# Attention with an output gate: one reciprocal of (1 + exp(-o)) times the denominator on VectorE, and the y transposes moved behind the q and k transposes

## The chip, the core and the metric

The kernel runs on one core of one Trainium2 chip. Its time is device microseconds from one launch, and the number that counts is the median over several runs. One profiled execution gives the trace from which every row below is taken.

## The reference, cut to what matters

Three layers follow one another. Attention is the layer that is touched; the others are only named.

```python
# attention, for each batch b (2), head h (8) and step t (768), head_dim 40:
m_new  = max(f_gate + m, i_gate)
C      = exp(f_gate + m - m_new) * C + exp(i_gate - m_new) * outer(v, k)
n      = exp(f_gate + m - m_new) * n + exp(i_gate - m_new) * k
h      = C @ q
denom  = max(abs(n . q), 1)
o      = 1 / (1 + exp(-o_gate))
y      = o * h / denom
# x = y as (1536 tokens, 320); an MLP 320 -> 2048 -> 320 with leaky relu;
# then 8 experts 320 -> 1024 -> 320, every token through all of them, weighted by a
# normalised gate (8 rounds over rows and columns)
```

## The kernel before

The 768 steps are cut into 6 chunks of 128, and a **unit** is one chunk of one batch with its 8 heads: 12 units, numbered n = 0 to 11, batch n % 2. Units 0 and 1 are written out ahead, units 2 and 3 in a short unrolled loop, units 4 to 11 in a hardware loop of four units each turn. Every engine has a queue of its own written by hand, in order, and engines wait for one another by semaphores only. What sets the order around the change is therefore the order of calls in each engine's loop body.

For unit n, by engine:

- TensorE: `exponents(n)` builds the gate exponents in PSUM (L1073 to L1080); `inter(n-1)` multiplies q by the state (L1106); `transposes(n)` turns q and k (L1089), once `ws_done` says that the weighted scores of unit n-1 were read, for they share a bank; `intra_and_state(n-1)` multiplies the weighted scores by v (L1118, it signals `y_prod`) and k by the weighted v (L1126); `scores(n)` (L1096). `y_transposes(n-2)` (L1136, L1137) turns the finished y into the layout of the MLP; it waits for `yy_done` of its unit, and for `xlo_done` of the unit before it, because all units use the same bank `yt_ps`.
- ScalarE: `out_gate(n)` takes exp(-o_gate) into `eo` (L540), `high_parts(n-2)` copies the high part of the transposed y (L547, L548), `exponentials(n)` (L555), `qk_copies(n)` (L561 to L564), and in the hardware loop `high_piece` (L580, L582), the high part of a piece of the first MLP weights.
- VectorE: `finish_y(n-1)` (L836 to L847) joins both products into `hh`, takes the denominator into `den`, its reciprocal (L843, 8 numbers a partition), multiplies by the gate into `ug` (L844) and by `hh` into `yy` (L847). Then `weigh(n)` (L814), `new_state(n-1)` (L856), `sigmoid(n)` (the reciprocal of 1 + exp, 320 numbers a partition, L867) and `low_parts(n-1)` (L821, L822), the low part of the transposed y. `weigh(n)` stands behind `finish_y(n-1)` in the queue, and `finish_y(n-1)` starts when `y_prod` of unit n-1 is there.
- GpSimd: `one_plus(n)` adds 1 to `eo` (L456; for units 0 and 1 VectorE does it, L863), then `pool_unit(n)` (L466, L472), and in the hardware loop `low_piece` (L310 to L318), the low part of a piece of the weights.

After the loops TensorE transposes y of unit 10, does `inter(11)`, a first hidden group of the MLP (L1211), `intra_and_state(11)`, a second hidden group, transposes y of unit 11, and goes on with the MLP.

Of the kernel before, what the change touches and what calls it, by code (L numbers as in the profile page):

```python
# [20 lines left out]
F32 = mybir.dt.float32  # L21
F32R = mybir.dt.float32r
BF16 = mybir.dt.bfloat16
ALU = mybir.AluOpType
# [4 lines left out]
def at_least(eng, sem, count):  # L29

    if isinstance(count, int) and count <= 0:
        return
    eng.wait_ge(sem, count)


def build(nc, q, k, v, i_gate, f_gate, o_gate, w_in, w_out, w_gate, w1, w2, out):
    P = 128
    B, H, S, D = q.shape
# [7 lines left out]
    NU = NC * B  # L46
# [23 lines left out]
    U_IT = 4  # L70
# [6 lines left out]
    with ctx:  # L77
# [3 lines left out]
        def sem(name):  # L81
            return ctx.enter_context(nc.semaphore(name))
# [33 lines left out]
        def asb(name, shape, dt):  # L116
            return sb(name, shape, dt, attn)
# [29 lines left out]
        eo = [asb(f"eo{b}", [P, DM], F32) for b in range(B)]  # L147
        t1 = asb("t1", [P, H, DV], F32)
        hh = asb("hh", [P, H, DV], F32)
        den = asb("den", [P, 2, H], F32)  # L150
        sg = asb("sg", [P, H, D], F32)
        ug = asb("ug", [P, H, D], F32)
        yy = [asb(f"yy{b}", [P, H, D], F32) for b in range(B)]
        attn.close()
# [76 lines left out]
        eo_done = sem("eo_done")  # L231
# [5 lines left out]
        yy_done = sem("yy_done")  # L237
# [1 line left out]
        FIN = 5  # L239
        wv_done = sem("wv_done")  # L240
        sd_done = sem("sd_done")
        e1_first = sem("e1_first")
        e1_done = sem("e1_done")
        sg_done = sem("sg_done")
        raw_in = sem("raw_in")
        RAW_IN = 5 * 16
        w_high = sem("w_high")
# [80 lines left out]
        def unit(i, j):  # L328

            n = 4 * i + j  # L330
            return n, 2 * i + j // 2, j % 2
# [57 lines left out]
        def _(pool):  # L389
# [57 lines left out]
            def alone():  # L447

                pool.sem_inc(pool_waits, 1)

            def one_plus(i, j):

                n, c, b = unit(i, j)
                pool.wait_ge(eo_done, n + 1)
                alone()
                pool.tensor_scalar(eo[b][:], eo[b][:], 1.0, None, ALU.add).then_inc(e1_done, 1)  # L456

            def pool_unit(i, j):

                n, c, b = unit(i, j)  # L460
# [38 lines left out]

            pool.wait_ge(gates_ok, 2)  # L500
            for j in range(2, U_IT):
                one_plus(0, j)
                pool_unit(0, j)

            pool.wait_ge(wg_in, 48)
# [2 lines left out]
            pool.tensor_tensor(wg[:, :, E:2 * E], wg_raw[:], wg[:, :, 0:E].bitcast(F32), ALU.subtract).then_inc(wg_step, 1)  # L508
            with pool.Fori(1, NU // U_IT) as i:
                for j in range(U_IT):  # L510
                    one_plus(i, j)
                    pool_unit(i, j)
                    low_piece(pool, 0, 0, (i - 1) * U_IT + j)

# [18 lines left out]
        def _(act):  # L533
            def out_gate(i, j):

                n, c, b = unit(i, j)
                act.wait_ge(unit_in[j], 80 * (i + 1))

                at_least(act, sg_done, n - 1)
                act.activation(eo[b][:], og[j][:], ACT.Exp, scale=-1.0).then_inc(eo_done, 1)  # L540

            def high_parts(i, j):

                m, c, b = unit(i, j)
                act.wait_ge(e_done, m + 1)
                tok = bass.ds(c * L + b * S, L)
                act.copy(xh[:, :, tok], yt_ps[:, 0:KT, :])  # L547
                act.copy(xr[0:DR, tok], yt_ps[0:DR, KT, :]).then_inc(xhi_done, 1)  # L548
# [17 lines left out]
            def act_unit(i, j):  # L566

                out_gate(i, j)
                high_parts(i, j - 2)
                exponentials(i, j)  # L570
                qk_copies(i, j)

            def high_piece(s, par, n):

# [167 lines left out]
        def _(dve):  # L742
# [82 lines left out]
            def finish_y(i, j):  # L825

                n, c, b = unit(i, j)
                done = FIN * n

                def fin(ins, k):  # L830
                    ins.then_inc(fin_step, 1)
                    dve.wait_ge(fin_step, done + k)

                dve.wait_ge(y_prod, n + 1)
                r_col = rw_t[:, bass.ds(c * 48 + b * H, H)]
                fin(dve.tensor_tensor(t1[:], heads(inter_ps)[:, :, 0:DV],  # L836
                                      r_col.unsqueeze(2).to_broadcast([P, H, DV]), ALU.mult), 1)
                dve.tensor_tensor(hh[:], heads(intra_ps)[:, :, 0:DV], t1[:], ALU.add).then_inc(ysum_read, 1)
                dve.wait_ge(ysum_read, n + 1)

                fin(dve.tensor_scalar(den[:, 1, :], hh[:, :, D], -1.0, 1.0, ALU.mult, ALU.max), 2)
                fin(dve.tensor_tensor(den[:, 0, :], hh[:, :, D], den[:, 1, :], ALU.max), 3)
                fin(dve.reciprocal(den[:, 1, :], den[:, 0, :]), 4)  # L843
                fin(dve.tensor_tensor(ug[:], sg[:], den[:, 1, :].unsqueeze(2).to_broadcast([P, H, D]), ALU.mult), 5)  # L844

                at_least(dve, e_done, n - 1)
                dve.tensor_tensor(yy[b][:], hh[:, :, 0:D], ug[:], ALU.mult).then_inc(yy_done, 1)  # L847
# [8 lines left out]
                    last = dve.tensor_tensor(st[b][rows, :, e, 0:DV], sp_v[rows, :, e, 0:DV], sd[b][rows, :, e, 0:DV], ALU.add)  # L856
                last.then_inc(st_done, 1)

            def sigmoid(i, j):
                n, c, b = unit(i, j)  # L860
                if isinstance(n, int) and n < 2:
                    dve.wait_ge(eo_done, n + 1)
                    dve.tensor_scalar(eo[b][:], eo[b][:], 1.0, None, ALU.add).then_inc(e1_first, 1)  # L863
                    dve.wait_ge(e1_first, n + 1)
                else:
                    dve.wait_ge(e1_done, n - 1)
                dve.reciprocal(sg[:], eo[b][:].rearrange("p (h d) -> p h d", d=D)).then_inc(sg_done, 1)  # L867
                dve.wait_ge(sg_done, n + 1)


            weigh(0, 0)
            rest_rows(1)
            sigmoid(0, 0)
            finish_y(0, 0)

            dve.wait_ge(rw_exp, 3)
# [10 lines left out]
                    last = dve.tensor_copy(decp[rows, 1:NC, b, :], dec_all[rows, 1:NC, b, :, half])  # L887
            last.then_inc(gates_ok, 1)
            new_state(0, 0)
            sigmoid(0, 1)  # L890
            low_parts(0, 0)
            for j in range(2, U_IT):
                finish_y(0, j - 1)
                weigh(0, j)
                new_state(0, j - 1)
                sigmoid(0, j)
                low_parts(0, j - 1)
            with dve.Fori(1, NU // U_IT) as i:
                for j in range(U_IT):
                    finish_y(i, j - 1)  # L900
                    weigh(i, j)
                    new_state(i, j - 1)
                    sigmoid(i, j)
                    low_parts(i, j - 1)
            finish_y(NU // U_IT, -1)

            def leak(u, f):
# [160 lines left out]
        def _(pe):  # L1068
# [105 lines left out]
            for j in range(2, U_IT):  # L1174
                if j == 2:
                    pe.wait_ge(parts_ok, 2)
                exponents(0, j)
                if j == 2:

                    pe.wait_ge(gates_ok, 2)  # L1180
                y_transposes(0, j - 2)
                inter(0, j - 1)
                transposes(0, j)
                intra_and_state(0, j - 1)
                scores(0, j)
            with pe.Fori(1, NU // U_IT) as i:
                for j in range(U_IT):
                    exponents(i, j)
                    y_transposes(i, j - 2)
                    inter(i, j - 1)  # L1190
                    transposes(i, j)
                    intra_and_state(i, j - 1)
                    scores(i, j)

# [185 lines left out]
```

## Time and profile before

| | us |
|---|---|
| median of 3 runs | 1015.48 (1014.93 to 1016.15) |
| the profiled execution | 1015.77 |
| its span | 1014.0 |
| TensorE busy | 982.8 (97%) |
| VectorE busy | 461.9 (46%) |
| ScalarE busy | 299.6 (30%) |
| GpSimd busy | 93.7 (9%) |

The span goes from the first to the last instruction of the profiled execution. Busy shares are means over all of it: attention takes the first 128 us, where VectorE is the busiest together with TensorE, and the MLP and experts the rest, where TensorE is. Units follow one another in attention, so a time per unit counts up to twelve times.

### The profile page before, as it was taken

The page shows a single profiled execution, that of the slowest core. Times are in us where ns is not written, and L with a number is a line of the kernel's source. Part 1 is how long each engine was busy: PE and PEld are TensorE (multiplying, and loading weights), DVE is VectorE, ACT ScalarE, POOL GpSimd, SP SyncE. Part 2 cuts the span into 40 slices and gives each one's busy share as a digit, 9 for nine tenths or more (in the row PEclk, how much of TensorE's full clock was granted, in tenths as well). Part 3 has the DMA queues.
Part 4 walks back from the last instruction along what each step waited for, and adds up shares of the span by engine and source line. Part 5 has one row for each costly group of instructions (what it writes and reads, how often), then busy time and mean ns, then how long its engine had stood idle before and what let it go on. Part 6 is the DMA issues. An engine that isn't in the chain of part 4 may idle for free.

```text
span 1014.0 us, 15373 instructions
## 1 busy us (share of the span) xinstructions
PE 982.8 (97%) x5500; PEld 867.2 (86%) x5500; DVE 461.9 (46%) x818; ACT 299.6 (30%) x571; POOL 93.7 (9%) x159
## 2 busy tenths in 40 slices
PE   5899899999999989999999999999999999999998
PEld 4788778888778978988999999899999998899997
DVE  8999956645553255244244223424423332442222
ACT  5555334434442221132122112312212221221111
POOL 7456400000000323000000000000000000000000
PEclk8999999999999999999999999999999999999999
DMA  9665210030030003003000300300120030000000
GB/s 153 122 84 74 72 43 1 0 114 1 1 99 17 1 1 114 1 1 109 6 0 0 114 1 0 114 0 0 34 80 0 0 114 0 0 0 0 26 26 26
DMA packets 67168, 39.19 MB, mean 39 GB/s; under 512 B 51488, under 2 KB 63264, under 8 KB 67136
## 3 DMA queue, kind: packets, MB, share of 16 engines
q1 hardware_dynamic: 67136, 38.78, 16.6%
q8 instruction: 18, 0.29, 0.1%
q14 instruction: 14, 0.11, 0.0%
HBM read 36.81 MB, written 1.97 MB: 38 GB/s over the span
## 4 chain that ended last, share of the span: by engine, by line
PE 89%; DVE 9%; issue 1%; DVEq 0%; ACT 0%; POOL 0%; POOLq 0%; ACTq 0%
PE psA L1211 43%; PE psB L1249 11%; PE psB L1251 11%; PE psB L1250 11%; PE psB L1227 2%; PE psB L1229 2%; PE psB L1228 2%; DVE sg L867 2%; PE psB L1234 1%; PE psB L1233 1%; DVE ug L844 1%; DVE ws L814 1%; PE psB L1118 1%; PE psA L1096 1%; DVE t L836 1%
## 5 line engine op out<-in xcount | busy, mean ns | idle before, releaser
L973 DVE SCALAR_TENSOR_TENSOR gl<-psA,gh 128x512 fp32r<-128x512 f32 x192 | 132.8, 692 | 341.2 <-ACT gh L708 341.1
L708 ACT ACTIVATE gh<-psA 128x512 fp32r<-128x512 f32 x192 | 115.0, 599 | 537.9 <-PE psA L1211 537.9
L1249 PE MATMUL psB<-w2s,gh 128*128 128x320 f32 x768 | 237.6, 309 | 0.0
L1250 PE MATMUL psB<-w2s,gh 128*128 128x320 f32 x768 | 237.3, 309 | 0.0
L1251 PE MATMUL psB<-w2s,gl 128*128 128x320 f32 x768 | 237.2, 309 | 0.0
L1211 PE MATMUL psA<-xh,w1h 128*128 (+1 forms) x480 | 190.6, 397 | 0.0
L1211 PE MATMUL psA<-xl,w1h 128*128 (+1 forms) x480 | 189.8, 395 | 0.0
L1211 PE MATMUL psA<-xh,w1l 128*128 (+1 forms) x480 | 189.1, 394 | 0.0
L1250 PEld LDWEIGHTS psB<-w2s,gh 128*128 128x128 f32 x768 | 144.3, 188 | 5.5
L1249 PEld LDWEIGHTS psB<-w2s,gh 128*128 128x128 f32 x768 | 144.2, 188 | 5.1
L1251 PEld LDWEIGHTS psB<-w2s,gl 128*128 128x128 f32 x768 | 144.4, 188 | 0.0
L1211 PEld LDWEIGHTS psA<-xl,w1h 128*128 128x128 f32 x480 | 90.3, 188 | 21.0
L1211 PEld LDWEIGHTS psA<-xh,w1h 128*128 128x128 f32 x480 | 90.4, 188 | 15.9
L1211 PEld LDWEIGHTS psA<-xh,w1l 128*128 128x128 f32 x480 | 90.4, 188 | 15.7
L1211 PE MATMUL psA<-xr,w1l 128*128 (+1 forms) x240 | 94.7, 394 | 0.0
L1211 PE MATMUL psA<-xr,w1h 128*128 (+1 forms) x240 | 94.2, 393 | 0.0
L1018 DVE SCALAR_TENSOR_TENSOR acc<-psB,pg,acc 128x320 f32 (+1 forms) x84 | 40.4, 544 | 97.5 <-PE psB L1251 97.5
L1211 PEld LDWEIGHTS psA<-xr,w1l 128*128 128x128 f32 x240 | 45.1, 188 | 10.9
L1211 PEld LDWEIGHTS psA<-xr,w1h 128*128 128x128 f32 x240 | 45.2, 188 | 10.3
L909 DVE SCALAR_TENSOR_TENSOR leaky<-hs 128x512 f32<-128x512 f32 x48 | 33.1, 691 | 43.2 <-ACT hs L646 43.0
L914 DVE TENSOR_TENSOR gl<-leaky,gh 128x512 fp32r<-128x512 f32 x48 | 33.2, 692 | 28.7 <-ACT gh L651 28.1
L646 ACT COPY hs<-psA 128x512 f32<-128x512 f32 x48 | 28.1, 586 | 58.6 <-PE psA L1211 53.8
(178 smaller groups left out, 970.6 us busy)
## 6 DMA issues: line engine op xcount, KB each, us to landing
raw<-in_moe_w_dram SPq DMA_DIRECT2D x16, 640.0 KB, 8.4
raw<-in_moe_w_dram SPq DMA_DIRECT2D x8, 1024.0 KB, 5.3
raw<-in_moe_w_dram SPq DMA_DIRECT2D x16, 256.0 KB, 6.1
raw<-in_moe_w_out_dram SPq DMA_DIRECT2D x4, 640.0 KB, 10.6
raw<-in_moe_w_in_dram SPq DMA_DIRECT2D x2, 1024.0 KB, 6.1
qs<-in_q_dram SPq DMA_DIRECT2D x12, 160.0 KB, 3.3
ks<-in_k_dram SPq DMA_DIRECT2D x12, 160.0 KB, 3.9
vz<-in_v_dram SPq DMA_DIRECT2D x24, 80.0 KB, 3.8
```

The costliest lines, as they stand in the source:

```text
L646: act.copy(hs[:, f % 2, :], h_ps[:, f % HB, :]).then_inc(hs_ok, 1)
L708: act.activation(gh[:, f % RING, :], h_ps[:, f % HB, :], ACT.Relu).then_inc(ghi_ok, 1)
L867: dve.reciprocal(sg[:], eo[b][:].rearrange("p (h d) -> p h d", d=D)).then_inc(sg_done, 1)
L909: dve.scalar_tensor_tensor(out=leaky[:, f % 2, :], in0=hs[:, f % 2, :], scalar=0.01, in1=hs[:, f % 2, :], op0=ALU.mult, op1=ALU.max).then_ ...
L914: dve.tensor_tensor(gl[:, f % RING, :], leaky[:, f % 2, :], gh[:, f % RING, :].bitcast(F32), ALU.subtract).then_inc(g_ready, 1)
L973: dve.scalar_tensor_tensor(out=gl[:, f % RING, :], in0=h_ps[:, f % HB, :], scalar=0.0, in1=gh[:, f % RING, :].bitcast(F32), op0=ALU.max, o ...
L1018: dve.scalar_tensor_tensor(out=dst, in0=y_ps[:, j, 0:DM], scalar=gate, in1=dst, op0=ALU.mult, op1=ALU.add).then_inc(o_read, 1)
L1211: last = pe.matmul(bank, lhs, rhs, start=n == 0, stop=n == total - 1)
L1227: pe.matmul(bank, wh, gh[:, slot, :], start=first, stop=False)
L1249: pe.matmul(bank, gh[:, slot, cols], W2S[par][:, f, 0, :], start=first, stop=False)
L1250: pe.matmul(bank, gh[:, slot, cols], W2S[par][:, f, 1, :], start=False, stop=False)
L1251: last = pe.matmul(bank, gl[:, slot, cols], W2S[par][:, f, 0, :], start=False, stop=end)
```

## The change

On VectorE `finish_y` now waits for `eo_done` of its unit, forms `dd = (eo + 1) * den` in one instruction, takes one reciprocal of its 320 numbers into `ug`, and multiplies by `hh` as before. The reciprocal of 8 numbers, the product `ug`, the whole of `sigmoid` with its call in each unit, and GpSimd's `one_plus` are gone, with three semaphores; ScalarE's `out_gate` waits for `yy_done` in place of `sg_done`. On TensorE `y_transposes(n-2)` moves behind `transposes(n)`, on ScalarE `high_parts(n-2)` behind `qk_copies(n)`, and on VectorE the low parts of a unit are taken one unit later.

```diff
--- before.py
+++ after.py
@@ -148,7 +148,7 @@
         t1 = asb("t1", [P, H, DV], F32)
         hh = asb("hh", [P, H, DV], F32)
         den = asb("den", [P, 2, H], F32)
-        sg = asb("sg", [P, H, D], F32)
+        dd = asb("dd", [P, H, D], F32)
         ug = asb("ug", [P, H, D], F32)
         yy = [asb(f"yy{b}", [P, H, D], F32) for b in range(B)]
         attn.close()
@@ -239,9 +239,6 @@
         FIN = 5
         wv_done = sem("wv_done")
         sd_done = sem("sd_done")
-        e1_first = sem("e1_first")
-        e1_done = sem("e1_done")
-        sg_done = sem("sg_done")
         raw_in = sem("raw_in")
         RAW_IN = 5 * 16
         w_high = sem("w_high")
@@ -448,13 +445,6 @@
 
                 pool.sem_inc(pool_waits, 1)
 
-            def one_plus(i, j):
-
-                n, c, b = unit(i, j)
-                pool.wait_ge(eo_done, n + 1)
-                alone()
-                pool.tensor_scalar(eo[b][:], eo[b][:], 1.0, None, ALU.add).then_inc(e1_done, 1)
-
             def pool_unit(i, j):
 
                 n, c, b = unit(i, j)
@@ -499,7 +489,6 @@
 
             pool.wait_ge(gates_ok, 2)
             for j in range(2, U_IT):
-                one_plus(0, j)
                 pool_unit(0, j)
 
             pool.wait_ge(wg_in, 48)
@@ -508,7 +497,6 @@
             pool.tensor_tensor(wg[:, :, E:2 * E], wg_raw[:], wg[:, :, 0:E].bitcast(F32), ALU.subtract).then_inc(wg_step, 1)
             with pool.Fori(1, NU // U_IT) as i:
                 for j in range(U_IT):
-                    one_plus(i, j)
                     pool_unit(i, j)
                     low_piece(pool, 0, 0, (i - 1) * U_IT + j)
 
@@ -536,7 +524,7 @@
                 n, c, b = unit(i, j)
                 act.wait_ge(unit_in[j], 80 * (i + 1))
 
-                at_least(act, sg_done, n - 1)
+                at_least(act, yy_done, n - 1)
                 act.activation(eo[b][:], og[j][:], ACT.Exp, scale=-1.0).then_inc(eo_done, 1)
 
             def high_parts(i, j):
@@ -566,9 +554,9 @@
             def act_unit(i, j):
 
                 out_gate(i, j)
-                high_parts(i, j - 2)
                 exponentials(i, j)
                 qk_copies(i, j)
+                high_parts(i, j - 2)
 
             def high_piece(s, par, n):
 
@@ -840,8 +828,11 @@
 
                 fin(dve.tensor_scalar(den[:, 1, :], hh[:, :, D], -1.0, 1.0, ALU.mult, ALU.max), 2)
                 fin(dve.tensor_tensor(den[:, 0, :], hh[:, :, D], den[:, 1, :], ALU.max), 3)
-                fin(dve.reciprocal(den[:, 1, :], den[:, 0, :]), 4)
-                fin(dve.tensor_tensor(ug[:], sg[:], den[:, 1, :].unsqueeze(2).to_broadcast([P, H, D]), ALU.mult), 5)
+                dve.wait_ge(eo_done, n + 1)
+                fin(dve.scalar_tensor_tensor(out=dd[:], in0=eo[b][:].rearrange("p (h d) -> p h d", d=D), scalar=1.0,
+                                             in1=den[:, 0, :].unsqueeze(2).to_broadcast([P, H, D]),
+                                             op0=ALU.add, op1=ALU.mult), 4)
+                fin(dve.reciprocal(ug[:], dd[:]), 5)
 
                 at_least(dve, e_done, n - 1)
                 dve.tensor_tensor(yy[b][:], hh[:, :, 0:D], ug[:], ALU.mult).then_inc(yy_done, 1)
@@ -856,21 +847,8 @@
                     last = dve.tensor_tensor(st[b][rows, :, e, 0:DV], sp_v[rows, :, e, 0:DV], sd[b][rows, :, e, 0:DV], ALU.add)
                 last.then_inc(st_done, 1)
 
-            def sigmoid(i, j):
-                n, c, b = unit(i, j)
-                if isinstance(n, int) and n < 2:
-                    dve.wait_ge(eo_done, n + 1)
-                    dve.tensor_scalar(eo[b][:], eo[b][:], 1.0, None, ALU.add).then_inc(e1_first, 1)
-                    dve.wait_ge(e1_first, n + 1)
-                else:
-                    dve.wait_ge(e1_done, n - 1)
-                dve.reciprocal(sg[:], eo[b][:].rearrange("p (h d) -> p h d", d=D)).then_inc(sg_done, 1)
-                dve.wait_ge(sg_done, n + 1)
-
-
             weigh(0, 0)
             rest_rows(1)
-            sigmoid(0, 0)
             finish_y(0, 0)
 
             dve.wait_ge(rw_exp, 3)
@@ -887,21 +865,18 @@
                     last = dve.tensor_copy(decp[rows, 1:NC, b, :], dec_all[rows, 1:NC, b, :, half])
             last.then_inc(gates_ok, 1)
             new_state(0, 0)
-            sigmoid(0, 1)
-            low_parts(0, 0)
             for j in range(2, U_IT):
                 finish_y(0, j - 1)
                 weigh(0, j)
                 new_state(0, j - 1)
-                sigmoid(0, j)
-                low_parts(0, j - 1)
+                low_parts(0, j - 2)
             with dve.Fori(1, NU // U_IT) as i:
                 for j in range(U_IT):
                     finish_y(i, j - 1)
                     weigh(i, j)
                     new_state(i, j - 1)
-                    sigmoid(i, j)
-                    low_parts(i, j - 1)
+                    low_parts(i, j - 2)
+            low_parts(NU // U_IT, -2)
             finish_y(NU // U_IT, -1)
 
             def leak(u, f):
@@ -1178,17 +1153,17 @@
                 if j == 2:
 
                     pe.wait_ge(gates_ok, 2)
-                y_transposes(0, j - 2)
                 inter(0, j - 1)
                 transposes(0, j)
+                y_transposes(0, j - 2)
                 intra_and_state(0, j - 1)
                 scores(0, j)
             with pe.Fori(1, NU // U_IT) as i:
                 for j in range(U_IT):
                     exponents(i, j)
-                    y_transposes(i, j - 2)
                     inter(i, j - 1)
                     transposes(i, j)
+                    y_transposes(i, j - 2)
                     intra_and_state(i, j - 1)
                     scores(i, j)
```

## Rows read from the trace of the kernel before

**Rows 1.** Chain of waits of the first 170 us, summed by line.
```profile
by line: PE psA L1211 14.1%; DVE sg L867 10.2%; issue 6.5%; DVE ug L844 6.0%; DVE ws L814 5.0%; PE psB L1118 4.2%; PE psA L1096 4.0%; PE psB L1227 3.1%; DVE t L836 3.0%; DVE hh L838 3.0%; PE psB L1228 3.0%; PE psB L1229 2.9%; DVE rest L793 
```

**Rows 2.** Timeline, VectorE, one unit: start, length (us), engine, line, operation, tiles.
```profile
65.51 0.50 DVE L836 TENSOR_TENSOR t<-psB,rw_t 128x328 f32<-128x328 f32 x1
...
66.58 0.27 DVE L841 TENSOR_SCALAR den<-hh 128x8 f32<-128x8 f32 x1
...
67.08 0.20 DVE L843 RECIPROCAL den<-den 128x8 f32<-128x8 f32 x1
67.32 1.14 DVE L844 TENSOR_TENSOR ug<-sg,den 128x320 f32<-128x320 f32 x1
68.49 0.62 DVE L847 TENSOR_TENSOR yy<-hh,ug 128x320 f32<-128x320 f32 x1
69.03 1.21 DVE L814 TENSOR_TENSOR ws<-psA,ex 128x1024 f32<-128x1024 f32 x1
70.16 0.66 DVE L856 TENSOR_TENSOR st<-psB,sd 64x164 f32<-64x164 f32 x2
70.85 2.15 DVE L867 RECIPROCAL sg<-eo 128x320 f32<-128x320 f32 x1
73.17 0.42 DVE L821 TENSOR_TENSOR xl<-psB,xh 128x256 f32 x1 [0.17 <-DVE sg L867]
...
73.92 0.50 DVE L836 TENSOR_TENSOR t<-psB,rw_t 128x328 f32<-128x328 f32 x1
```

**Rows 3.** Timeline, TensorE, the same unit.
```profile
70.41 0.60 PE L1089 MATMUL psA<-ident,qs 128*128 128x128 f32 x4
...
71.29 1.92 PE L1118 MATMUL psB<-vz,ws 128*128 128x96 f32 x16
...
73.94 1.98 PE L1096 MATMUL psA<-qt,kt 128*128 128x128 f32 x16
```

**Rows 4.** Timeline, ScalarE and GpSimd, the same unit and the next.
```profile
68.07 1.25 POOL L456 TENSOR_SCALAR eo<-eo 128x320 f32<-128x320 f32 x1
...
70.11 0.26 ACT L548 CAST xr<-psB 64x128 f32 x1
...
73.16 0.51 ACT L580 CAST w1h<-raw  x1
...
74.25 1.00 POOL L310 TENSOR_TENSOR w1l<-raw,w1h  x1 [2.43 <-ACT w2s L582]
...
75.39 0.32 POOL L316 TENSOR_TENSOR w2r<-raw,w2s  x1
...
75.68 0.86 POOL L318 TENSOR_TENSOR w2s<-raw,w2s  x1
```

**Rows 5.** View of tile ug: times are min/median/max in ns.
```profile
L844 DVE TENSOR_TENSOR ug<-sg,den x12: 492/1134/1137, 32.3 to 126.5; 128x320 f32<-128x320 f32 x12
```

**Rows 6.** Timeline, VectorE and GpSimd, unit 1 finished and unit 2 weighed.
```profile
41.41 0.50 DVE L836 TENSOR_TENSOR t<-psB,rw_t 128x328 f32<-128x328 f32 x1 [1.15 <-PE psB L1118]
...
42.97 1.13 POOL L466 TENSOR_TENSOR wv<-vz,rw_t 128x164 f32<-128x164 f32 x2
43.12 0.66 DVE L844 TENSOR_TENSOR ug<-sg,den 128x320 f32<-128x320 f32 x1
...
44.37 1.21 DVE L814 TENSOR_TENSOR ws<-psA,ex 128x1024 f32<-128x1024 f32 x1
```

**Rows 7.** Busy time by stage: stretch, length, engines, granted clock, DMA share, GB/s.
```profile
30.00:36.00 6.00, 2.10 (x15) 1.49 (x16) 5.85 (x11) 1.44 (x3) 4.16 (x5) 0.92 0.97 212
```

**Rows 8.** Timeline of the last unit and the start of the MLP.
```profile
119.58 1.22 DVE L814 TENSOR_TENSOR ws<-psA,ex 128x1024 f32<-128x1024 f32 x1
...
119.72 0.44 PE L1136 MATMUL psB<-ident,yy 128*128 128x128 f32 x2 [1.56 <-DVE yy L847]
...
124.80 0.50 DVE L836 TENSOR_TENSOR t<-psB,rw_t 128x328 f32<-128x328 f32 x1 [0.36 <-PE psB L1118]
...
127.59 0.44 PE L1136 MATMUL psB<-ident,yy 128*128 128x128 f32 x2 [0.95 <-DVE yy L847]
```

## The prediction

> **What bounds the kernel now.** I read the page first, for which engine fills which part. TensorE is busy nearly throughout, and what the MLP and the experts take is untouched. So the question is when attention, whose last y is transposed at 127.59 us [rows 8], hands over. Next the chain of waits of the first 170 us, summed by line [rows 1]: outside the MLP's own lines the largest shares are VectorE's sigmoid reciprocal (10.2%) and the product `ug` (6.0%). Then VectorE's timeline of one unit [rows 2]: from one `t` to the next, 65.51 to 73.92, it never idles longer than the 0.17 us ahead of `xl`. A unit takes 8.43 us: the weighing starts at 69.03 in unit 5 and at 119.58 in unit 11 [rows 2, 8], 50.55 us for six units.
>
> The reader must then see a second thing in the same rows, in which order the waits end. Let T be the end of a weighing, 69.03 + 1.21 = 70.24. TensorE turns q and k from 70.41 and multiplies by v from 71.29 to 73.21 [rows 3]; before that nothing exists that `finish_y` could work on. VectorE fills just that gap: state to 70.82, sigmoid reciprocal to 73.00, low parts to 73.9, `t` at 73.92 = T + 3.68 [rows 2]. The reciprocal of 2.15 us is on the chain by the order of the queue, but TensorE would have held VectorE until T + 2.97 without it. Thus it costs 0.7 us of critical time there, not 2.15.
>
> The loop that must not grow is: weighing, turn q and k, multiply by v, `finish_y`, next weighing, since `weigh(n)` is queued behind `finish_y(n-1)`. Scores are no part of it: they begin at 73.94 and end at 75.92, the weighing they feed starts 8.43 us after 69.03, at 77.46 [rows 2, 3].
>
> **The change part by part, in a unit of the hardware loop.** All from T.
>
> Moved low parts and y transposes. Behind the weighing VectorE has state (to T + 0.58) and then low parts, 0.75 us with their gaps (73.17 to 73.92 [rows 2]): T + 1.35. They belong to unit n-3, whose high parts are long copied, so they don't wait. But the y transposes of n-2 write the bank that these low parts read, so TensorE, which has turned q and k by about T + 1.0, waits for T + 1.40. The transposes take about 0.4 us (0.44 for two matmuls [rows 8], the third overlapping), and the product with v is queued behind them: it starts at T + 1.8 in place of 1.05, ends 1.92 later at 3.7 [rows 3], and `t` starts at T + 3.75. That is 0.07 later than now, though VectorE has dropped 2.15 us from this gap: the reciprocal's absence turns into idle time of 2.4 us, from T + 1.35 to 3.75. The transposes' old wait for `yy` goes, but it was no delay: it lay beside the weighing.
>
> `finish_y`. `t` and `hh` take 1.07 with gaps (65.51 to 66.58 [rows 2]). The first `den` instruction took 0.27 and ended at 66.85, when GpSimd's `w1l` piece, which in this pattern starts 0.33 us behind `t` (74.25 beside 73.92) and runs 1.00, ended at 66.84 [rows 2, 4]: VectorE waits for GpSimd there. After the change that piece is later, since ScalarE copies the high parts of y, two copies of 0.26 and about as much, 0.5 us together, ahead of the weight piece of 73.16 [rows 4]: GpSimd starts at T + 4.01 + 0.5 less the 0.05 by which q and k are turned sooner, T + 4.45, and ends at 5.45. `den` wants to start at 3.75 + 1.07 = 4.82 and so ends at 5.5; bounds: 5.0 without the meeting, 5.5 with it. The second `den` instruction is 0.2 (66.88 to 67.08 by the start of the next row [rows 2]): T + 5.7.
>
> Out go the small reciprocal (0.24 from its start to the next) and `ug`; in comes `dd`. The trace has no `(a + 1) * b` over 128x320; the nearest row is `ug` itself, same operands and size, 0.492 at best and 1.137 where GpSimd is at work [rows 5]. The 1.14 arose beside the `w2s` piece: `ug` of 67.32 ended at 68.46, GpSimd's piece at about 68.1 [rows 2, 4]. In unit 2 `ug` was issued between the first and second of two GpSimd products and needed only 0.66 while GpSimd's pair stretched to 1.13 [rows 6], so VectorE gets in between two GpSimd instructions. `dd` at T + 5.7 falls on the 0.32 us piece ahead of `w2s`. I take 0.55; bounds 0.49, and 1.4 if it lands behind `w2s` (0.86 + 0.49, [rows 4, 5]). The wait for `eo_done` costs nothing: that exponential is made a unit earlier. Then the reciprocal over 320 numbers, 2.15 + 0.03: the same shape as the one removed. It goes to T + 8.45. `yy` follows; `weigh` starts 0.54 behind the start of `yy` (68.49 to 69.03 [rows 2]), about 0.41 when `yy` isn't stretched by `one_plus`, which is gone: T + 8.9.
>
> Sum: 3.75 to `t`, 5.15 from `t` to the weighing (before 3.52, 65.51 to 69.03), and 1.21: **10.1 us a unit in place of 8.43**. The 2.15 us moved from a stretch where TensorE's latency covered them into the one stretch that nothing covers.
>
> What else is removed: `sigmoid` 2.15 and its gap of 0.17, off the gap as said; `one_plus`, 1.25 us on GpSimd [rows 4], which waits 2.43 us for ScalarE in each unit anyway [rows 4], so nothing but the shorter `yy` counted above. The semaphores go with them. No DMA moves: the loads of a slot wait for `d_done` and `eo_done`, both earlier than needed.
>
> The whole. Start: unit 0 loses its sigmoid and its y transposes are out of the way of unit 1's products; by the order of the queues I get `t` of unit 1 1.1 us earlier than 41.41, at 40.3 (bounds: no gain, and 2.15). From there units 1 and 2 have no weight pieces beside them: 4.6 us from `t` to the weighing (1.07 + 0.4 + 0.52 + 2.18 + 0.41), so the weighing of unit 2 starts at 44.9 (now 44.37 [rows 6]); then 3.75 + 4.6 + 1.21 = 9.56 to unit 3 at 54.5, and 10.1 for each of units 4 to 11: 135.3 against 119.58 [rows 8], **+15.7**.
>
> The end: after the last weighing (T = 120.80 now) TensorE transposes y of unit 10 at 119.72, before T, because `yy` was enough. Now it waits for low parts to T + 1.40. What follows up to `t` of unit 11 took 124.80 - 119.72 = 5.08 [rows 8], so `t` is at T + 6.48 in place of 4.00. `finish_y` to the transposes of unit 11 took 2.79 (124.80 to 127.59); now 1.07 + 0.4 + 0.52 + 2.18 + 0.49 + 0.05 = 4.71. Together 11.19 against 6.79: **+4.4**. TensorE has only one hidden group of about 1.9 us to lay over it.
>
> Total 15.7 + 4.4 = 20.1. Behind attention TensorE is full, so nothing takes it back. The profiled execution's own 1015.77 (span 1014.0) becomes 1035.9; against the median, 1015.48, that is **1035.6**.
>
> **The rivals.** *One unit's VectorE work is the bound, and it shrinks (faster).* VectorE fills the unit, and by sums it loses 0.24, 0.17 and 0.65 (1.14 to 0.49), 1.06 of 8.43 us. If the 2.15 were as well covered as now, eight units give 8.5 and the start 1.1: 1006. It decides in this kernel by whether `weigh(n)` can pass `finish_y(n-1)`; it can't, as one queue holds both, and `t` needs the product with v. Even with no meeting of any kind and y transposes free, the loop is 2.9 + 4.6 + 1.21 = 8.7, above 8.43. The Trainium skill, "VectorE: DVE Perf Modes", section "Rules for kernel authors", advises for chained VectorE instructions to minimise their count, not their semaphores; this change takes one off each unit's chain, and by that rule alone the case here would come true. The rows above bear it out only as far as VectorE never idles. I give it 3 in 100, and no change 1.
>
> *VectorE and GpSimd don't meet.* `den` ends at T + 5.0 and `dd` takes 0.49: 9.56 a unit throughout, 8 times 0.55 less: 1031. For: pieces move with ScalarE, whose copies I place to a few tenths only. 21 in 100.
>
> *`dd` lands behind `w2s`.* 0.86 more in eight units: 1042.5. For: `ug` does just that now. Against: `dd` is issued 0.24 earlier in the row of pieces. 15 in 100.
>
> *TensorE's clock falls.* A unit leaves TensorE idle for some 2.2 us in one piece, and 2.8 at the end. In the trace it waits 1.56 us ahead of 119.72 [rows 8] with no drop, while in the stretch of 30 to 36 us, where it was busy for 2.10 of 6.00, the granted clock shows 0.92 [rows 7]. At the lower of the two levels, 1.2 against 2.4 GHz, the 3 us of TensorE work between T and `t` would take up to twice as long: 1045 to 1065 by how many units are hit. The Trainium skill, "TensorE: Matmul & The Clock Gate", section "Why this matters for your kernels", warns of idle gaps between bursts that send the clock back; by it this rival would be likelier the longer the gap. 8 in 100.
>
> **How the numbers follow.** Main case 52 in 100, with 1033 to 1039 for itself. The range of 1029 to 1044 takes in the second and third rivals and the bounds of the start, and leaves out the fall of the clock and the gain. What a measurement can tell is about 0.2%, 2 us: faster 0.03, the same 0.01, slower 0.96.
>
> **What would show it.** Right: from `t` to `ws` about 5.1 us and from `ws` to `t` about 5.0; VectorE idle for over 2 us ahead of `t`, released by the product with v; y transposes released by `xr` of the low parts; the last weighing near 135 us. `den` of nearly 0.7 us shows the meeting with `w1l`. Wrong: `t` to `ws` under 4 us, or a `dd` over 0.7, or a granted clock below 1.00 in 50 to 130 us. The forecast falls as a whole if VectorE's idle time ahead of `t` is missing.

## The result, and the profile after

The changed kernel is slower: 1042.61 us (median of 4 runs, 1041.67 to 1043.82) against 1015.82, a ratio of 1.0264 (95% interval 1.0247 to 1.0282), 26.8 us. The forecast was 1035.6, slower, with a range of 1029 to 1044.

The page of the changed kernel, its span and the busy time of each engine (us, share, instructions):

```profile
span 1040.1 us, 15320 instructions
...
PE 992.2 (95%) x5489; PEld 874.3 (84%) x5500; DVE 452.1 (43%) x804; ACT 299.8 (29%) x571; POOL 83.9 (8%) x149
```

VectorE does 9.8 us less work than before and GpSimd 9.8 less, and the kernel is 26 us longer. So the time is not in the sum of what these two engines do. TensorE is busy for 9.4 us more with the same work, which fits the falls of its clock shown below. VectorE's timeline of one unit of the hardware loop after the change, as [rows 2] show it before (start, length in us, engine, line, operation, tiles; in brackets the idle time ahead and what ended it):

```profile
87.85 1.22 DVE L802 TENSOR_TENSOR ws<-psA,ex 128x1024 f32<-128x1024 f32 x1
88.98 0.66 DVE L847 TENSOR_TENSOR st<-psB,sd 64x164 f32<-64x164 f32 x2
89.67 0.42 DVE L809 TENSOR_TENSOR xl<-psB,xh 128x256 f32 x1
90.11 0.28 DVE L810 TENSOR_TENSOR xr<-psB,xr 64x128 f32 x1
92.98 0.50 DVE L824 TENSOR_TENSOR t<-psB,rw_t 128x328 f32<-128x328 f32 x1 [2.58 <-PE psB L1093]
...
94.04 0.48 DVE L829 TENSOR_SCALAR den<-hh 128x8 f32<-128x8 f32 x1
...
94.76 0.54 DVE L832 SCALAR_TENSOR_TENSOR dd<-eo,den 128x320 f32<-128x320 f32 x1
95.33 2.15 DVE L835 RECIPROCAL ug<-dd 128x320 f32<-128x320 f32 x1
97.52 0.49 DVE L838 TENSOR_TENSOR yy<-hh,ug 128x320 f32<-128x320 f32 x1
97.93 1.22 DVE L802 TENSOR_TENSOR ws<-psA,ex 128x1024 f32<-128x1024 f32 x1
```

The unit is 97.93 - 87.85 = 10.08 us. The reader is to see two things: the bracket at `t`, 2.58 us idle until TensorE's product with v (L1093) was there, and the reciprocal of 2.15 us behind it, between `t` and the next weighing. From `t` to the weighing it takes 4.95 us, before 3.52.

TensorE and GpSimd in the same unit, which answer to [rows 3] and [rows 4]:

```profile
90.54 0.41 PE L1111 MATMUL psB<-ident,yy 128*128 128x128 f32 x2 [0.26 <-DVE xr L810]
...
90.90 1.92 PE L1093 MATMUL psB<-vz,ws 128*128 128x96 f32 x16
...
93.50 0.99 POOL L307 TENSOR_TENSOR w1l<-raw,w1h  x1 [2.86 <-ACT w2s L570]
...
94.91 1.11 POOL L315 TENSOR_TENSOR w2s<-raw,w2s  x1
...
99.30 0.63 PE L1064 MATMUL psA<-ident,qs 128*128 128x128 f32 x4 [1.97 <-DVE ws L802]
```

The y transposes wait for `xr` of the low parts, the product with v starts at 90.90, 1.83 us behind the weighing's end at 89.07 (before 1.05), and ahead of the next q and k transposes TensorE is idle for 1.97 us.

That idle time is the second part of the result. Five stretches of 2 us of the changed kernel (length, then busy time of PE, PEld, DVE, ACT, POOL with instructions, granted clock, DMA share, GB/s), and below them the end of attention as in [rows 8]:

```profile
48.00:50.00 2.00, 2.00 (x11) 1.96 (x10) 0.00 (x0) 1.66 (x5) 0.19 (x1) 0.50 0.00 0
58.00:60.00 2.00, 2.00 (x10) 2.00 (x11) 1.11 (x4) 1.07 (x2) 0.83 (x1) 0.50 0.04 8
90.00:92.00 2.00, 1.74 (x17) 1.53 (x15) 0.38 (x2) 1.83 (x5) 0.64 (x1) 1.00 0.00 0
110.00:112.00 2.00, 2.00 (x11) 1.96 (x10) 0.64 (x2) 0.99 (x3) 0.83 (x1) 0.50 0.00 0
142.00:144.00 2.00, 2.00 (x10) 1.97 (x11) 0.58 (x2) 0.53 (x2) 0.00 (x0) 0.50 0.99 234
```

```profile
139.24 1.22 DVE L802 TENSOR_TENSOR ws<-psA,ex 128x1024 f32<-128x1024 f32 x1
...
141.94 0.66 PE L1111 MATMUL psB<-ident,yy 128*128 128x128 f32 x2 [5.10 <-DVE xr L810]
...
149.25 0.50 DVE L824 TENSOR_TENSOR t<-psB,rw_t 128x328 f32<-128x328 f32 x1 [5.13 <-PE psB L1093]
...
153.99 0.69 PE L1111 MATMUL psB<-ident,yy 128*128 128x128 f32 x2 [2.90 <-DVE yy L838]
```

Four of the five show 0.50, the lower of the clock's two levels, with TensorE fully busy. Where it stays at 1.00, a unit of the hardware loop takes 10.09 us. Where it falls, `t` comes later behind the end of the weighing: 5.4 us in unit 2, 5.1 in unit 3 and 5.0 in unit 8, against 3.9 in units 4 to 7, 9 and 10; and in unit 11 8.8, where the forecast had 6.5. The y of unit 11 is transposed at 153.99, before at 127.59 [rows 8]: 26.4 us, the whole difference. From there on both kernels take 886 us to their end.

### The profile page after: what moved, and what is told of

The parts are those of the page before. It is cut to its first block, busy times and chain, and to the rows that moved or that the text cites. A ratio compares the mean times of both kernels' runs of the same rounds, so it can differ in the third digit from the quotient of the medians.

```text
span 1040.1 us, 15320 instructions
## 1 busy us (share of the span) xinstructions
PE 992.2 (95%) x5489; PEld 874.3 (84%) x5500; DVE 452.1 (43%) x804; ACT 299.8 (29%) x571; POOL 83.9 (8%) x149
## 3 DMA queue, kind: packets, MB, share of 16 engines
HBM read 36.81 MB, written 1.97 MB: 37 GB/s over the span
## 4 chain that ended last, share of the span: by engine, by line
PE 88%; DVE 9%; issue 2%; DVEq 0%; ACT 0%; POOL 0%; POOLq 0%; ACTq 0%
PE psA L1186 42%; PE psB L1224 11%; PE psB L1226 11%; PE psB L1225 11%; DVE ug L835 2%; PE psB L1093 2%; PE psB L1202 2%; PE psB L1204 2%; PE psB L1203 2%; PE psB L1209 1%; PE psB L1208 1%; DVE dd L832 1%; PE psA L1064 1%; DVE hh L826 1%; DVE t L824 1%
```

## Experiments

Each was timed beside the kernel before on one chip; the ratio is to that. The column "unit" is the usual distance from one weighing to the next in the hardware loop at granted clock 1.00.

| run | unit, us | time, us | ratio (95% interval) |
|---|---|---|---|
| before | 8.43 | 1015.8 to 1016.5 | |
| the change | 10.09 | 1042.61 | 1.0264 (1.0247 to 1.0282) |
| e1 fusion only | 9.66 | 1036.21 | 1.0209 (1.0176 to 1.0243) |
| e2 move only | 8.86 | 1022.85 | 1.0066 (1.0044 to 1.0089) |
| e3 change, no reciprocal | 9.12 | 1023.78 | 1.0073 (1.0051 to 1.0095) |
| e5 change, TensorE kept busy | 10.09 | 1038.75 | 1.0220 (1.0197 to 1.0244) |
| e4 before, no sigmoid reciprocal | 8.43 | 1013.43 | 0.9970 (0.9958 to 0.9981) |
| e6 before, weight pieces gated | 7.55 | 1008.44 | 0.9928 (0.9910 to 0.9946) |
| e7 tanh | 8.43 | 1013.47 | 0.9968 (0.9954 to 0.9982) |
| e8 tanh and gate | 7.42 | 1006.36 | 0.9893 (0.9873 to 0.9913) |
| e9 fusion, gated and filled | 8.94 | 1027.29 | 1.0111 (1.0090 to 1.0131) |

### The two halves of the change

**e1**, the changed kernel with the three orders put back:

```diff
-                    inter(i, j - 1)
-                    transposes(i, j)
                     y_transposes(i, j - 2)
+                    inter(i, j - 1)
+                    transposes(i, j)
...
-                    low_parts(i, j - 2)
+                    low_parts(i, j - 1)
```

> Only the fusion: one product and one reciprocal in finish_y, no sigmoid, no one_plus, but y transposes, high parts and low parts in the order of before. Theory A (the 2.15 us reciprocal has moved from the gap that TensorE's transposes and product with v cover into the loop weighing, product with v, finish_y, next weighing, and the moved y transposes add a wait of 0.7 us to that loop): t comes about 3.0 us behind a weighing's end in place of 3.8, a unit of the hardware loop takes about 9.6 us (before 8.43, the whole change 10.09), the last weighing stands near 130 us, and the time is 1028 to 1033. Rival B (the move of the y transposes is what costs, the fusion is free or better, since VectorE has 1.06 us less to do in a unit): a unit of 7.4 to 8.4 us, and a time of 1007 to 1016.

The unit is 9.66 us, as theory A said to a tenth, and rival B falls: the fusion by itself makes the kernel slower. The time is 3 us above what I wrote, since the clock falls here too. A unit where TensorE stayed at 1.00 and the next (VectorE's `t` and `den`, TensorE's transposes of q):

```profile
79.21 0.50 DVE L824 TENSOR_TENSOR t<-psB,rw_t 128x328 f32<-128x328 f32 x1 [1.79 <-PE psB L1093]
...
80.28 0.85 DVE L829 TENSOR_SCALAR den<-hh 128x8 f32<-128x8 f32 x1
...
84.53 1.22 DVE L802 TENSOR_TENSOR ws<-psA,ex 128x1024 f32<-128x1024 f32 x1
...
84.67 0.44 PE L1111 MATMUL psB<-ident,yy 128*128 128x128 f32 x2 [2.03 <-DVE yy L838]
...
86.67 1.06 PE L1064 MATMUL psA<-ident,qs 128*128 128x128 f32 x4
...
90.52 0.50 DVE L824 TENSOR_TENSOR t<-psB,rw_t 128x328 f32<-128x328 f32 x1 [3.44 <-PE psB L1093]
...
95.81 1.22 DVE L802 TENSOR_TENSOR ws<-psA,ex 128x1024 f32<-128x1024 f32 x1
```

Behind an idle time of 2.03 us the transposes of q take 1.06 in place of 0.60, and `t` comes 4.8 us behind the weighing's end in place of 3.1. Units 4, 6 and 9 of this run were so, and the clock fell at its end too (0.57 from 136 to 140 us). `den` takes 0.85: with `t` earlier, it meets nearly the whole `w1l` piece on GpSimd, which started at 80.10 and took 1.00.

**e2**, the kernel before with only the orders of the change, and low parts ahead of the sigmoid:

```diff
                     new_state(i, j - 1)
+                    low_parts(i, j - 2)
                     sigmoid(i, j)
-                    low_parts(i, j - 1)
...
-                    y_transposes(i, j - 2)
                     inter(i, j - 1)
                     transposes(i, j)
+                    y_transposes(i, j - 2)
```

> Only the move: y transposes behind the q and k transposes, high parts behind the q and k copies, low parts one unit later and ahead of the sigmoid, which stays with its reciprocal, the small reciprocal, the product and one_plus. Theory A: the product with v waits for low parts and y transposes, but the sigmoid (2.15 us) now fills that time, so t is only 0.1 us later from a weighing's end; the weight pieces on GpSimd come 0.45 us later and hold den and ug a little longer; a unit takes 8.5 to 8.9 us. At the end y transposes of unit 10 wait about 2.6 us longer, with an idle TensorE of about 4 us and then a lower granted clock, 2 to 5 us in all. Time 1019 to 1025. Rival B (the move is what costs 1.7 us a unit): a unit near 10 us and 1033 to 1042.

As theory A had it: 8.86 us a unit. The end costs most of the rest in the trace: TensorE waits for low parts there, the clock falls to 0.50, and `t` of unit 11 comes 8.1 us behind the last weighing, before 4.0. (The traced execution took 1024.48, 1.6 us above the median, so its end may be costlier than the usual one.) So the move costs 0.43 us a unit alone (8.43 to 8.86) and 0.43 on top of the fusion (9.66 to 10.09); the fusion costs 1.23 either way. The halves add up. On top of the fusion the 0.43 is a difference of two: `t` comes 3.91 us behind the weighing's end in place of 3.12, and the way from `t` to the next weighing falls from 5.32 to 4.95, because `den` then meets less of the `w1l` piece.

### The reciprocal itself

**e3**, in the changed kernel, and **e4**, in the kernel before:

```diff
-                fin(dve.reciprocal(ug[:], dd[:]), 5)
+                fin(dve.tensor_tensor(ug[:], dd[:], hh[:, :, 0:D], ALU.add), 5)
```

```diff
-                dve.reciprocal(sg[:], eo[b][:].rearrange(...)).then_inc(sg_done, 1)
+                dve.tensor_scalar(sg[:], eo[b][:].rearrange(...), 1.0, None, ALU.mult).then_inc(sg_done, 1)
```

> The changed kernel with the reciprocal of dd left out: an addition of dd and hh of the same size stands in its place, so y is not the reference's. Theory A: finish_y gets shorter by 2.15 less 0.5 to 0.6, about 1.6 us, and since nothing covers it each unit gets shorter by just that: 10.09 becomes about 8.4 to 8.5 us; twelve units give 19 to 20 us, and TensorE's idle stretches shrink so that some of the lost clock comes back: 1016 to 1023. Rival B (y transposes behind low parts set the pace): a unit stays over 9.5 us, time over 1035.

> The kernel before with the reciprocal of the sigmoid left out (a multiplication by 1.0 of the same size in its place, so y is not the reference's). Theory A (the 2.15 us of the sigmoid lie in a gap of VectorE's critical chain that TensorE's product with v holds open anyway): t can come only 0.7 us sooner, and most of that is eaten by GpSimd's weight pieces, which start by ScalarE's clock: den waits for the piece of 1.00 us and ug for the one of 0.86, so a unit is 8.3 to 8.4 us in place of 8.43 and the time 1012 to 1017. Rival B (VectorE is the bound of a unit, each of its instructions counts): 1.8 us a unit, 995 to 1000.

In e4 the unit stays at 8.43, with 1.8 us of VectorE's work gone from each: in the hardware loop the sigmoid's reciprocal cost nothing. Of the 3 us of the run 1.7 are there when unit 4 is weighed (58.91 for 60.59), before the weight pieces begin, and none is added up to unit 11 (117.86 for 119.58). The other 1.3 us are no more than the spread of what follows attention, which took 884.8 to 886.5 us in the traces of all these kernels. In e3 the unit falls to 9.12, by 0.97 and not by the 1.6 that I wrote, and the time of 1023.78 is just above the 1016 to 1023 expected. The rows show what took the reciprocal's place, e4's first (VectorE, and the piece on GpSimd), then e3's:

```profile
75.77 1.21 DVE L814 TENSOR_TENSOR ws<-psA,ex 128x1024 f32<-128x1024 f32 x1
...
80.11 0.50 DVE L836 TENSOR_TENSOR t<-psB,rw_t 128x328 f32<-128x328 f32 x1 [1.31 <-PE psB L1118]
...
80.99 1.00 POOL L310 TENSOR_TENSOR w1l<-raw,w1h  x1 [2.39 <-ACT w2s L582]
...
81.18 0.84 DVE L841 TENSOR_SCALAR den<-hh 128x8 f32<-128x8 f32 x1
...
82.49 1.14 DVE L844 TENSOR_TENSOR ug<-sg,den 128x320 f32<-128x320 f32 x1
```

```profile
83.09 0.54 DVE L832 SCALAR_TENSOR_TENSOR dd<-eo,den 128x320 f32<-128x320 f32 x1
...
83.66 1.03 DVE L835 TENSOR_TENSOR ug<-dd,hh 128x320 f32<-128x320 f32 x1
...
84.72 0.63 DVE L838 TENSOR_TENSOR yy<-hh,ug 128x320 f32<-128x320 f32 x1
85.28 1.21 DVE L802 TENSOR_TENSOR ws<-psA,ex 128x1024 f32<-128x1024 f32 x1
```

In e4 `t` is 3.13 us behind the weighing's end in place of 3.68, and `den` then stands still for 0.84 until the `w1l` piece ends, in place of 0.27 [rows 2]. In e3 the addition with two tiles takes 1.03 where the same size takes 0.49 alone, and `yy` 0.63, beside GpSimd. GpSimd's pieces start by ScalarE's pace: `w1l` begins 5.22 us behind the start of the weighing in e4 (80.99 - 75.77) as in the kernel before (74.25 - 69.03 [rows 2, 4]), though `t` came sooner. What VectorE does not spend in the reciprocal it spends waiting for the pieces. For e3 this means that the instruction put in the reciprocal's place was itself held up, so its 0.97 us is less than what the reciprocal alone costs.

### The clock

**e5**: small products whose results nobody reads, called fillers below: 24 ahead of each unit's q and k transposes and, at the end, 70 and 40 ahead of the y transposes of units 10 and 11 (these two calls are not shown).

```diff
+            def filler(count, bank=None):
+                bank = psB[:, 1, HP * VP:512] if bank is None else bank
+                for _ in range(count):
+                    pe.matmul(bank, warm_up[:, 0:P], warm_up[:, 0:P], start=True, stop=True)
...
             def transposes(i, j):
+                if not (isinstance(n, int) and n < 2):
+                    filler(24)
```

> The changed kernel with 24 small bf16 products of 128 columns, whose results nobody reads, ahead of each unit's q and k transposes, 70 ahead of the y transposes of unit 10 and 40 ahead of those of unit 11: they stand where TensorE is idle (2.0 us a unit, 5.1 and 2.9 at the end). Theory C (the steady unit of 10.09 us is what the working gave, and the 7 us beyond the forecast of 1035.6 are the three stretches at granted clock 0.50, at 48 to 52 and 58 to 61 us, at 110 to 112, and from 140 us): the granted clock stays at 1.00 from 40 us on, the unit stays at 10.1 everywhere, and the time falls to 1035 to 1038. Rival D (those units are long because of their own waits, the clock is a by-product): the clock rises and the time stays at 1041 to 1044.

```profile
52.00:60.00 8.00, 7.16 (x77) 6.62 (x77) 6.66 (x11) 2.48 (x5) 1.75 (x3) 1.00 0.62 85
...
110.00:120.00 10.00, 9.05 (x94) 8.50 (x93) 7.24 (x12) 4.35 (x10) 4.20 (x7) 1.00 0.00 0
...
140.00:150.00 10.00, 9.35 (x85) 8.32 (x86) 5.46 (x10) 1.70 (x4) 0.00 (x0) 1.00 0.63 192
```

From 44 us on the clock is at 1.00, the units are 10.0 to 10.2 throughout, and `t` of unit 11 comes 6.52 us behind the weighing: the forecast had 6.48. The ratio falls from 1.0264 to 1.0220: 22.3 us above the kernel before (1016.44 on this chip), where the change was 26.8 above and the forecast without a fall of the clock was 20.1. The time of 1038.75 is a little above my 1035 to 1038. One part is the fillers' own: `t` of unit 1 is at 41.31 and not at 39.97, since 24 fillers stand ahead of it in TensorE's queue and take 2.18 us at 36.12, where the clock is low in both kernels (0.62 from 36 to 38 us). From `t` of unit 1 to `t` of unit 11 the changed kernel takes 109.28 us and e5 103.73. These 5.55 us are what the falls of the clock cost behind 40 us.

### The fused loop with nothing around it, and the meetings with GpSimd

**e9** is e1 with the gate of e6 and 24 fillers ahead of each unit's y transposes. **e6** is one line in the kernel before:

```diff
+                    pool.wait_ge(yy_done, 4 * i + j)
                     low_piece(pool, 0, 0, (i - 1) * U_IT + j)
```

> The fusion alone, as in the run with only the fusion, with every cost around it taken away: GpSimd's weight pieces start when yy is done, and 24 small bf16 products that nobody reads stand ahead of each unit's y transposes, so that TensorE is not idle while VectorE forms the reciprocal. Theory A: what stays is the loop itself, 3.1 us from a weighing's end to t, 4.6 from t to the next weighing, 1.22 for the weighing: 8.9 us a unit at granted clock 1.00, above the 8.43 of before, and with the later start of the MLP (+1.9 us in finish_y of unit 11, +1.2 for the last weight piece) 1022 to 1028. Rival B (it was the clock and the meetings with GpSimd that made the fused form slow): a unit of 8.4 us or less and a time of 1010 to 1017.

> The kernel before, but GpSimd begins the weight piece of unit n only when yy of unit n-1 is done, that is beside VectorE's weighing, state and sigmoid, which read PSUM or one tile and were never stretched, in place of beside den and ug. Theory E (the meeting with GpSimd costs 0.65 us in ug, 0.1 in den and 0.1 in yy per unit): ug takes 0.49 to 0.55, a unit 7.6 to 7.8 us, where TensorE's own work of the unit is the next bound; the last weight piece is 1.2 us later for the first hidden group; 1009 to 1013. Rival: the stretched ug is no part of what ends last, time 1015 to 1018.

e9 gives 8.94 us a unit with the clock at 1.00 from 44 to 120 us and `den`, `dd` and `yy` at their shortest (0.17, 0.49, 0.49): with clock and meetings out of the way the fused form is still above the 8.43 of before. Rival B falls. (At the very end of attention, 130 to 132 us, the clock fell to 0.50 in e9 too; the unit is free of that, the time is not.) e6 gives 7.55, a little better than the 7.6 to 7.8 expected, and is 0.72% faster than the kernel before, at 1008.44 for the 1009 to 1013 expected. So with the same gate in both, the fusion costs 1.39 us a unit (7.55 to 8.94). `ug` in e6, and where the piece has gone:

```profile
72.32 0.17 DVE L842 TENSOR_SCALAR den<-hh 128x8 f32<-128x8 f32 x1
...
72.96 0.49 DVE L845 TENSOR_TENSOR ug<-sg,den 128x320 f32<-128x320 f32 x1
...
73.90 1.22 DVE L815 TENSOR_TENSOR ws<-psA,ex 128x1024 f32<-128x1024 f32 x1
...
74.28 1.00 POOL L310 TENSOR_TENSOR w1l<-raw,w1h  x1 [2.63 <-DVE yy L848]
```

`ug` is 0.49 in place of 1.14 and `den` 0.17 in place of 0.27. VectorE still forms the sigmoid's reciprocal while TensorE multiplies by v, as before, and the piece on GpSimd now runs beside the weighing.

### A faster version

**e7** replaces the sigmoid by (1 + tanh(o/2)) / 2, so that `sigmoid` and `one_plus` go as in the change (not shown in the lines below); **e8** adds the gate of e6 to it:

```diff
-                act.activation(eo[b][:], og[j][:], ACT.Exp, scale=-1.0).then_inc(eo_done, 1)
+                act.activation(eo[b][:], og[j][:], ACT.Tanh, scale=0.5).then_inc(eo_done, 1)
...
+                fin(dve.scalar_tensor_tensor(out=ug[:], in0=eo[b][:]..., scalar=1.0, in1=den[:, 1, :]...,
+                                             op0=ALU.add, op1=ALU.mult), 5)
...
+                dve.scalar_tensor_tensor(out=yy[b][:], in0=hh[:, :, 0:D], scalar=0.5, in1=ug[:],
+                                         op0=ALU.mult, op1=ALU.mult).then_inc(yy_done, 1)
```

> The kernel before with no reciprocal over 320 numbers at all: ScalarE takes tanh(o/2) in place of exp(-o), ug = (tanh + 1) * reciprocal(den), yy = (hh * 0.5) * ug; sigmoid and one_plus are gone. Theory A: VectorE loses 2.3 us a unit, but in the gap, so t comes 0.7 us sooner and den and ug then wait for the weight pieces: 8.2 to 8.4 us a unit, 2 us gained at unit 0: 1010 to 1014. Rival B (VectorE's sum): 7.4 us a unit or less and 1003 to 1007.

> The tanh form and the gated weight pieces together. Theory A with E: both covers are gone, t comes about 3.0 us behind a weighing, t to weighing takes 2.6 to 2.9 us, and a unit is bound by TensorE at 7.4 to 7.7 us: 1006 to 1010, the fastest of all. If the gain of the two is no more than that of the gate alone, 1010 to 1013, TensorE was already the bound with the gate.

e7 takes out the large reciprocal and GpSimd's `one_plus`, and the unit is still 8.43, as in e4: it is the pieces that hold it. What it gains comes ahead of them: in the trace unit 4 is weighed 4.9 us earlier (55.73 in place of 60.59), and unit 11 still 4.9. With the gate too the unit is 7.42 and the time 1006.36, the fastest here, 1.07% below the kernel before. Both runs are within what theory A expected. TensorE is the bound there, but so it is in e6 already. One stretch of e6, then two of e8:

```profile
60.00:70.00 10.00, 9.95 (x93) 9.66 (x93) 9.48 (x17) 6.71 (x14) 7.37 (x14) 1.00 0.84 98
```

```profile
60.00:70.00 10.00, 9.95 (x93) 9.75 (x94) 5.97 (x15) 6.54 (x14) 5.03 (x9) 1.00 0.63 78
...
90.00:100.00 10.00, 9.95 (x93) 9.75 (x94) 6.25 (x16) 6.22 (x13) 4.72 (x9) 1.00 0.01 1
```

TensorE is busy for 9.95 of 10.00 us in both, before for 8.47 in this stretch. Most of the gain is the gate's (8.0 of the 10.1 us by the medians). Removing the reciprocal on top of it pays 2.1 us and 0.13 a unit, and without the gate 3.0 us and nothing a unit: in either case most of it is gained at the start.

## Why the prediction was right, and what it mis-sized

**The loop.** Right. It said 10.1 us a unit, built of 3.75, 5.15 and 1.21; measured are 3.91, 4.95 and 1.22, so two small misses cancel. Where the reciprocal stood it cost 0.7 us of critical time by the forecast, and nothing by e4, since the meetings with GpSimd take that too; the fusion costs 1.23 (e1).

**The moved low parts and y transposes.** Right as a mechanism, 0.07 us forecast against the 0.23 that `t` came later, and idle time of 2.4 against 2.58. But the forecast compared with the old kernel only; against the fusion alone the move costs 0.43 us a unit (e1), which its sum contains and no sentence named.

**`den` and `dd`.** Right: `dd` 0.54 for 0.55, `den` 0.48 for 0.68: the piece on GpSimd stood where placed (4.43 us behind the weighing's end for 4.45), and `t` was 0.16 late. Neither the rival without meetings (9.56 a unit) nor the one with `dd` behind `w2s` came about; in the latter's place the `w2s` piece took 1.11 in place of 0.86, so here GpSimd waited. The Trainium skill, "SBUF — State Buffer", section "SBUF: two separate sides", says that of a VectorE instruction with two inputs in SBUF and a GpSimd instruction that reads SBUF the one that starts first holds the ports they share for its whole length, and the other waits. The trace agrees in the order: `dd` started at 94.76 and `w2s` at 94.91. In the size it agrees roughly: `dd` then had 0.39 us to run, and `w2s` took 0.25 longer.

**The start.** `t` of unit 1 at 39.97 for 40.3, the weighing of unit 2 at 45.03 for 44.9. That these agree is partly luck: the forecast had 4.6 us from `t` to the weighing in units 1 and 2, and they took 5.06 and 4.96.

**The end.** The step said 11.19 us from the last weighing's end to the y transposes of unit 11; it took 13.53. `finish_y` was right (4.74 for 4.71). What failed is the step that what follows the y transposes, up to `t` of unit 11, takes the old 5.08 us: it took 7.3, as TensorE, idle for 5.10 us, came back at granted clock 0.50. In e5, with the clock at 1.00, it took 5.04.

**The clock.** This is the term that was mis-sized. The sum has nothing for it. It was a rival with 8 in 100, in place of the main case and at 1045 us or more; it came true on top of the main case and cheaper, in four places. In units 2, 3, 8 and 11 `t` came 1.6, 1.2, 1.1 and 2.3 us later behind the weighing than in e5, where the clock stayed up. A little of that came back between `t` and the next weighing, for a later `t` meets less of the `w1l` piece (4.78 in unit 8 for 4.96), and 5.55 us is left. The forecast had named idle times of 2.2 us a unit and 2.8 at the end, but overlooked the longest, 5.1 us ahead of the y transposes of unit 10, though its own working placed them at T + 1.40 and the last scores long before. With 5.55 us it would have read 1041.2 against 1042.61; some 0.8 of the rest is the 5.06 and 4.96 named under the start.

**The range.** That 1042.61 lies in 1029 to 1044 is in part luck. The main case had 1033 to 1039 for itself. The range went up to 1044 for the rival with `dd` behind `w2s`, which did not happen, and was said to leave out the fall of the clock, which did. A granted clock below 1.00 in 50 to 130 us was among the signs of being wrong, and it was there (0.50 at 58 to 60 and 110 to 112 us). The last weighing came at 139.24 and not near 135, for the same reason. The other signs of being right came: 4.95 us from `t` to the weighing, 5.13 from the weighing to `t`, 2.58 us idle ahead of `t` behind the product with v, and y transposes released by `xr`.

**The rival of VectorE's sum.** Refuted three times: e4 takes 1.8 us off VectorE's work in a unit and e7 more, with no change of the unit, and e1 takes some off, with one instruction fewer a unit, and is 1.23 us a unit longer.

Not settled is which idle time makes the clock fall. The length alone does not decide it: in the changed kernel 1.97 us of idle time ahead of 99.30 left it at 1.00, while 1.86 us ahead of 57.99 and 2.06 ahead of 109.47 did not, and in e1 it fell behind 2.03 us at 84.67 and not behind 2.08 at 96.03. The Trainium skill, "TensorE: Matmul & The Clock Gate", section "Why this matters for your kernels", warns of idle gaps between bursts of matmuls, but of longer ones than these; here the clock fell behind 1.86 us, and the measurement decides.

## What to carry to other kernels

Before an instruction is merged into another, ask which wait covered it. Here 2.15 us of reciprocal cost nothing in a unit beside a matmul group, and the fusion that put it behind that group's result cost 1.2 us a unit, though the engine's total work fell. Then look at what a removed instruction was hiding: in e3, e4 and e7 the next thing in line, GpSimd's pieces, took two fifths of what was removed or all of it. The one-line gate that moved those pieces gained 8.0 us, where removing the reciprocal gained 2.1 on top. And where a change leaves TensorE idle for about 2 us in every round, as here, put a price on a fall of its clock in the main case and not in a rival only.

## What the runs showed of the hardware that was not expected

- The granted clock fell to 0.50 behind idle times of 1.9 to 2.1 us, in some units and not in others of the same kernel with nearly the same idle time. Matmuls that took 0.60 us for a group of four took 1.06 there. In e5, with 1.5 us of fillers in each of these idle times, it stayed at 1.00 from 44 us on.
- VectorE's reciprocal over 128x320 took 2152 to 2154 ns in all twelve units of the changed kernel, whatever GpSimd did beside it, while the product `ug` of the same size took 492 to 1137 ns before [rows 5]. That it reads one tile only is not shown to be the reason: the first `den` instruction reads one tile too, and took 0.17 alone and 0.85 beside `w1l` (e1). With the reciprocal in place `yy` behind it took 0.49 in the units with pieces, while in e3, with an addition there, it took up to 0.63.
